# Two 64-row matmuls, one in each half of the array, for the low weights of the last 64 channels of product one

## What is computed

```python
w = np.exp(weight - weight.max(-1, keepdims=True)); w /= w.sum(-1, keepdims=True) + 1e-9
x = einsum('hk,bskhg->bshg', w, last_7_tokens(x_pad)).reshape(8192, 192)
h = x @ w_in_1;  x = (h / (1 + np.exp(-h))) @ w_out_1                      # layer one
h = x @ w_in_2;  out = np.where(h > 0, h, np.exp(np.minimum(h, 0)) - 1) @ w_out_2   # layer two
```

## Time and profile before

| | |
|---|---|
| median of the runs | 1193.97 us |
| span of the profiled execution | 1191.4 us |
| TensorE matmul busy | 1167.8 us, 98% |
| TensorE weight load busy | 964.3 us, 81% |
| VectorE busy | 880.6 us, 74% |
| ScalarE busy | 454.8 us, 38% |
| GpSimd busy | 64.9 us, 5%, all before 130 us |
| matmuls | 5130, of which 10 warm up |

### The profile page before, as it was taken

How to read it: one execution, slowest core, us unless ns; L and a number is a source line. 1 busy time by engine, 2 the same in 40 slices (tenths; PEclk the granted TensorE clock), 3 DMA queues, 4 the chain that set the end, 5 groups by cost and what they waited for, 6 DMA issues and landing times.

```text
span 1191.4 us, 12698 instructions
## 1 busy us (share of the span) xinstructions
PE 1167.8 (98%) x5130; PEld 964.3 (81%) x5130; DVE 880.6 (74%) x1023; ACT 454.8 (38%) x499; POOL 64.9 (5%) x57
## 2 busy tenths in 40 slices
PE   4999999999999999999999999999999999999998
PEld 3788888888888888888888888888888888888886
DVE  6999647679977745677997764676898775577676
ACT  5243334444423234444433232444443222354443
POOL 6444100000000000000000000000000000000000
PEclk8999999999999999999999999999999999999999
DMA  4321000000010000000100000000011000000000
GB/s 146 96 65 32 18 1 1 14 15 14 19 32 18 19 1 1 1 14 14 32 14 18 19 18 1 1 14 1 14 32 32 1 1 1 1 1 14 14 1 26
DMA packets 16843, 22.94 MB, mean 19 GB/s; under 512 B 1424, under 2 KB 9616, under 8 KB 16784
## 3 DMA queue, kind: packets, MB, share of 16 engines
q1 hardware_dynamic: 16784, 22.13, 6.2%
HBM read 15.83 MB, written 6.29 MB: 19 GB/s over the span
## 4 chain that ended last, share of the span: by engine, by line
PE 96%; DVE 3%; DMA 0%; issue 0%; ACT 0%; SPq 0%; ACTq 0%; DVEq 0%
PE hid L504 48%; PE acc L528 19%; PE acc L531 19%; PE acc L530 10%; DVE mix L375 1%; DVE mix L338 1%; DVE glo L429 1%; DMA xT<-x_rows 0%; DVE ghi L441 0%; DVE mix L371 0%; ACT ghi L291 0%; DVE mix L335 0%; DVE x L355 0%; DVE g L453 0%; ACT g L299 0%
## 5 line engine op out<-in xcount | busy, mean ns | idle before, releaser
L504 PE MATMUL hid<-x,wi 128*128 128x512 f32 x2560 | 623.1, 390 | 6.2 <-DVE x L355 6.2
L504 PEld LDWEIGHTS hid<-x,wi 128*128 128x128 f32 x2560 | 481.4, 188 | 106.8 <-DVE x L355 6.6
L299 ACT ACTIVATE g<-hid 128x1024 f32<-128x1024 f32 x256 | 263.4, 1029 | 712.0 <-PE hid L504 696.0
L429 DVE TENSOR_TENSOR glo<-g,ghi 128x1024 fp32r<-128x1024 f32 x256 | 319.1, 1247 | 31.7 <-ACT ghi L291 30.3
L441 DVE CAST ghi<-g 128x1024 fp32r<-128x1024 f32 x128 | 91.5, 714 | 150.5 <-ACT g L299 150.1
L528 PE MATMUL acc<-glo,wo 128*128 128x512 f32 x512 | 199.5, 390 | 2.5 <-DVE glo L429 2.5
L528 PE MATMUL acc<-ghi,wo 128*128 128x512 f32 x512 | 199.4, 390 | 1.2 <-ACT ghi L291 0.9
L531 PE MATMUL acc<-glo,wo 128*128 128x512 f32 x512 | 199.2, 389 | 0.0
L530 PE MATMUL acc<-ghi,wo 128*128 128x512 f32 x512 | 199.2, 389 | 0.0
L531 PE MATMUL acc<-ghi,wo 128*128 128x512 f32 x512 | 199.2, 389 | 0.0
L449 DVE TENSOR_SCALAR g<-g 128x1024 f32<-128x1024 f32 x128 | 88.7, 693 | 117.8 <-ACT g L299 117.2
(11 more groups left out here) (39 smaller groups left out, 212.6 us busy)
## 6 DMA issues: line engine op xcount, KB each, us to landing
xT<-x_rows SPq DMA_DIRECT2D x16, 518.0 KB, 4.2
stg<-w_in SPq DMA_DIRECT2D x16, 256.0 KB, 3.2
outT<-stg SPq DMA_DIRECT2D x16, 256.0 KB, 2.0
stg<-w_out SPq DMA_DIRECT2D x16, 192.0 KB, 3.3
outT<-tail SPq DMA_DIRECT2D x16, 128.0 KB, 2.3
tap<-tap_rows SPq DMA_DIRECT2D x1, 7.0 KB, 1.7
```

The costliest lines, as they stand in the source:

```text
L299: eng.activation(g[:, u % 2, :], hid[u % 2][:, :], fn).then_inc(s_fn, 1)
L429: eng.tensor_tensor(glo[:, u % NG, :], g[:, u % 2, :], ghi[:, u % NG, :].bitcast(F32), ALU.subtract).then_inc(s_glo, 1)
L504: last = eng.matmul(hid[u % 2][:, t * TOK:(t + 1) * TOK], w[:, j, wk, t * P:(t + 1) * P], xs[:, xk, :], start=n == 0, stop=n == len(plan) - 1)
```

## The change

The two full matmuls of the pair (3, 2) become two matmuls of 64 rows: tile t = 0 with the low weights on partitions 0 to 63, tile t = 1 with those on partitions 64 to 127. Both have the high part of x as the moving operand, which must therefore stand on both halves. A new tile `x1d` (layer one) or `x2d` (layer two) holds the second copy of it. For even chunks `x[:, 2]` has the high part on 0 to 63 and the copy lies on 64 to 127; for odd chunks it is the other way round, so that an even and an odd chunk share a copy tile.

```diff
-        wi = [sb(f"wi{l}", [P, NPAIR, 4, PW], F32R) for l in range(2)]
+        wi = [sb(f"wi{l}", [P, NPAIR, 3 * PW + P], F32R) for l in range(2)]
...
+        x1d = sb("x1d", [P, TOK], F32R)
+        x2d = sb("x2d", [P, GROUP // 2, TOK], F32R)
...
+        LOW, HIGH = slice(0, REST), slice(REST, P)
+
+        def hi_rows(c):
+            return HIGH if c % 2 else LOW
...
             def first_matmul(u):
...
-                plan = [(0, 0), (0, 1), (2, 0), (1, 2), (3, 2)]
+                plan = [(0, 0), (0, 1), (2, 0), (1, 2)]
                 for n, (wk, xk) in enumerate(plan):
...
                     for t in range(2):
-                        last = eng.matmul(hid[u % 2][:, t * TOK:(t + 1) * TOK],
-                                          w[:, j, wk, t * P:(t + 1) * P], xs[:, xk, :],
-                                          start=n == 0, stop=n == len(plan) - 1)
+                        eng.matmul(hid_t[t], w[:, j, wk * PW + t * P:wk * PW + (t + 1) * P], xs[:, xk, :],
+                                   start=n == 0, stop=False)
+                if c == 0:
+                    eng.wait_ge(s_wlo, POOL_OPS * (l * NPAIR + j) + 3)
+                for t, rows in enumerate((LOW, HIGH)):
+                    mv = xs[rows, 2, :] if rows == hi_rows(c) else xd[rows]
+                    last = eng.matmul(hid_t[t], w[rows, j, 3 * PW:3 * PW + P], mv, start=False, stop=True)
                 last.then_inc(s_hid, 1)
```

On GpSimd the one subtraction of a piece's input weights becomes three, and on VectorE one operation is added to the averaging of each chunk (19 steps for 18) and one to `split_result`:

```diff
-                eng.tensor_tensor(wi[l][:, j, 2:4, :].rearrange("p a n -> p (a n)"), stg_in(q),
-                                  wi[l][:, j, 0:2, :].rearrange("p a n -> p (a n)").bitcast(F32),
-                                  ALU.subtract).then_inc(s_wlo, 1)
+                eng.tensor_tensor(wi[l][:, j, 2 * PW:3 * PW], stg_in(q)[:, 0:PW],
+                                  wi[l][:, j, 0:PW].bitcast(F32), ALU.subtract).then_inc(s_wlo, 1)
+                for t, rows in enumerate((LOW, HIGH)):
+                    cols = slice(PW + t * P, PW + (t + 1) * P)
+                    if t:
+                        eng.wait_ge(s_wlo, POOL_OPS * q + 2)
+                    eng.tensor_tensor(wi[l][rows, j, 3 * PW:3 * PW + P], stg_in(q)[rows, cols],
+                                      wi[l][rows, j, cols].bitcast(F32), ALU.subtract).then_inc(s_wlo, 1)
...
-                eng.tensor_copy(xs[:, 2, :], tail[:, :]).then_inc(s_x2, 1)
-                eng.wait_ge(s_x2, 3 * rank(s) - 1)
-                eng.tensor_tensor(xs[REST:P, 2, :], tail[REST:P, :], xs[REST:P, 2, :].bitcast(F32),
-                                  ALU.subtract).then_inc(s_x2, 1)
+                eng.tensor_copy(xd[low], tail[low, :]).then_inc(s_x2, 1)
+                eng.tensor_copy(xs[high, 2, :], tail[high, :]).then_inc(s_x2, 1)
+                eng.wait_ge(s_x2, X2_OPS * rank(s) - 2)
+                eng.tensor_tensor(xs[low, 2, :], tail[low, :], xd[low].bitcast(F32), ALU.subtract)\
+                   .then_inc(s_x2, 1)
```

More of the change, by code:

```diff
@@ L81, in mixed_two_layer_ffn @@
     conv_start[1], conv_len[1] = 0, NPAIR - 2
-    CONV_OPS = 2 * NTAP + 4
+    CONV_OPS = 2 * NTAP + 5
+    POOL_OPS = 5
+    X2_OPS = 4
     POOL_TAPS = 5
@@ L187, in load_piece, with lo_rows, x_of, dup_of @@
                .then_inc(done, 16)
+        LOW, HIGH = slice(0, REST), slice(REST, P)
+        def hi_rows(c):
+            return HIGH if c % 2 else LOW
+        def lo_rows(c):
+            return LOW if c % 2 else HIGH
+        def x_of(l, c):
+            return x2[:, c % GROUP, :, :] if l else x1[:, c % 2, :, :]
+        def dup_of(l, c):
+            return x2d[:, c % GROUP // 2, :] if l else x1d[:, :]
         block = ctx.enter_context(nc.Block())
@@ L279, in _ @@
             eng.wait_ge(s_tap, 7)
[L280 to L283, removed]
+            eng.wait_ge(s_mix0, MIX0_STEPS - 1)
+            eng.activation(x1[:, 0, 0, :], mix[:, 0, :], ACT.Copy, scale=tstat[:, 4:5]).then_inc(s_hi0, 1)
+            eng.wait_ge(s_mix0, MIX0_STEPS)
+            eng.activation(x1d[HIGH, :], mix[HIGH, 1, :], ACT.Copy, scale=tstat[HIGH, 5:6]).then_inc(s_hi0, 1)
+            eng.activation(x1[LOW, 0, 2, :], mix[LOW, 1, :], ACT.Copy, scale=tstat[LOW, 5:6]).then_inc(s_hi0, 1)
             for q in range(2, NSTG):
@@ L350, in _ @@
             eng.wait_ge(s_tap, 7)
[L351 to L357, removed]
+            eng.wait_ge(s_hi0, 1)
+            eng.scalar_tensor_tensor(x1[:, 0, 1, :], mix[:, 0, :], tstat[:, 4:5], x1[:, 0, 0, :].bitcast(F32),
+                                     ALU.mult, ALU.subtract).then_inc(s_lo0, 1)
+            eng.wait_ge(s_hi0, 2)
+            eng.scalar_tensor_tensor(x1[HIGH, 0, 2, :], mix[HIGH, 1, :], tstat[HIGH, 5:6],
+                                     x1d[HIGH, :].bitcast(F32), ALU.mult, ALU.subtract).then_inc(s_lo0, 1)
             def conv_op(c, i):
@@ L366, in conv_op @@
                         eng.wait_ge(s_lo0, 2)
-                        eng.wait_ge(s_hi0, 2)
+                        eng.wait_ge(s_hi0, 3)
                     else:
@@ L377, in conv_op @@
                 else:
-                    xs = x1[:, c % 2, :, :]
+                    xs, xd = x_of(0, c), dup_of(0, c)
+                    high, low = hi_rows(c), lo_rows(c)
+                    r0, r1 = tstat[:, 4:5], tstat[:, 5:6]
                     if i == 2 * NTAP and c >= 2:
@@ L413, in split_result @@
             def split_result(s):
-                a, xs = acc[s % 2], x2[:, chunk(s) % GROUP, :, :]
+                c = chunk(s)
+                a, xs, xd = acc[s % 2], x_of(1, c), dup_of(1, c)
+                high, low = hi_rows(c), lo_rows(c)
                 eng.wait_ge(s_first1, rank(s))
@@ L493, in first_matmul @@
                         eng.wait_ge(s_fn, u - 1)
-                xs = x1[:, c % 2, :, :] if l == 0 else x2[:, c % GROUP, :, :]
-                w = wi[l]
-                plan = [(0, 0), (0, 1), (2, 0), (1, 2), (3, 2)]
+                xs, xd, w = x_of(l, c), dup_of(l, c), wi[l]
+                hid_t = [hid[u % 2][:, t * TOK:(t + 1) * TOK] for t in range(2)]
+                plan = [(0, 0), (0, 1), (2, 0), (1, 2)]
                 for n, (wk, xk) in enumerate(plan):
                     if c == 0 and n == 2:
-                        eng.wait_ge(s_wlo, 3 * (l * NPAIR + j) + 1)
+                        eng.wait_ge(s_wlo, POOL_OPS * (l * NPAIR + j) + 1)
                     if u == 0 and n == 3:
                         eng.wait_ge(s_lo0, 2)
+                        eng.wait_ge(s_hi0, 3)
                     for t in range(2):
-                        last = eng.matmul(hid[u % 2][:, t * TOK:(t + 1) * TOK],
-                                          w[:, j, wk, t * P:(t + 1) * P], xs[:, xk, :],
-                                          start=n == 0, stop=n == len(plan) - 1)
+                        eng.matmul(hid_t[t], w[:, j, wk * PW + t * P:wk * PW + (t + 1) * P], xs[:, xk, :],
[5 more added lines that the diff above has]
+                    last = eng.matmul(hid_t[t], w[rows, j, 3 * PW:3 * PW + P], mv, start=False, stop=True)
                 last.then_inc(s_hid, 1)
@@ L536, in _ @@
             eng.wait_ge(s_whi, 1)
[L537 removed]
+            warm = wi[0][:, 0, 0:TOK]
             for i in range(WARM):
```

32 lines of the change are left out of this document (18 added, 14 removed).

## The result

The changed kernel takes 1241.9 us, the median of 4 runs (1241.29 to 1242.03), against 1193.99 of before: 1.0401 times as long, with an interval of 1.0386 to 1.0416. The profiled execution has a span of 1239.5 us, 48.1 more than before. I had forecast 1151.5 and a range to 1228; it is 4% slower.

The account below looks back on a forecast made before the run. TensorE's matmul slots were taken to bound the kernel: 232 units x 0.2267 = 52.6 us saved, minus 7 and 3, left 42.6, so a span of 1148.8 and a median of 1151.5 us; range 1138 to 1228.

Parts of the forecast that it names:

- What bounds the kernel: Whole kernel: TensorE's 5,120 matmuls of 0.2267 us make 1160.5 of the 1191.4 us; VectorE stands close behind in some stages.
- I take 'together': Each unit's pair: loads hidden, both 64-row matmuls stream at once, 0.2267 us saved a unit, 52.6 in 232 units; chance 0.40.
- The row I leaned on: TensorE at 35.45 after a wait: an exposed weight load, the next load starting at 35.56, so 0.11 us a load.
- the emptying with loads held back: At each change of matmul form the array must empty and two loads a unit are exposed: 1275 us; chance 0.12.
- The variant with loads ahead: The array empties at each change of matmul form, 0.324 us paid a unit, but loads stay hidden: 1224 us; chance 0.18.
- My break-even: A pause of about 98 ns at each change between full and half matmuls, (52.6 - 7) / 464, decides gain or loss.
- The term of 7 us for stages 0 to 2: VectorE sets the pace there: stages 1 and 2 4.7 us longer, stage 0 2.7 longer, nothing saved in 24 units.
- the price of 0.37 us of VectorE for each microsecond of GpSimd: Stages 1 and 2: 11.2 us of VectorE lost to 30.3 of GpSimd; 15.0 more GpSimd means 5.6 more VectorE.
- Stages 7, 15 and 23: VectorE needs 35.9 us in stages that would be 34.45; 1 us each comes back as waits, 3 in all.
- 0.34 for slower: Chance given to the changed kernel being slower than before, against 0.61 for faster and 0.05 for the same.

Follow-up runs that it names:

- 19 slots: The changed kernel with one full matmul in place of the two half ones, one tile's low weights left out: 1136.78 us, 0.952 of before.
- the kernel with the cut alone: The kernel before, with GpSimd's 512-element subtraction cut by columns into 256, 128 and 128 and TensorE's wait split: 1190.71 us, 0.9975 of before.

## Why the prediction was wrong, point by point

**What bounds the kernel** was right: TensorE alone sets the steady stages, 36.27 then and 37.89 now. But "only fewer or shorter matmul slots, or a stall, can move the end" passed over the stretch ahead of the first product, 19.85 us long, at whose end TensorE waits for VectorE: the other engines' edits made it 1.4 us shorter, and the sum had no term for it.

**The step that failed** is "I take 'together'", with a load of 0.11 hidden in the slot before and nothing lost at the passage. The pair's loads do go out together (within 0.01 us) and the pair does share a slot, which the kernel with both halves on the same partitions shows. But the loads go out only 0.09 us after the slot of the full matmul ahead, 0.32 after its start, where a full load starts with it; and the next full load goes out in the same way behind the pair. That they wait for the array to empty is my reading of these times, and the short half matmuls, which leave both gaps as they are, agree with it. The row I leaned on the earlier trace rows gave the price of an exposed load rightly, 0.11. What it could not give is that both changes of form expose one.

**The rival that came true** is the emptying with loads held back, at 0.12, given 1275. Its mechanism is the measured one; its size was too high, because I took the empty stretch from the end of a matmul's record, 0.162, and it is 0.09. With the measured terms a unit loses 2 x (0.09 + 0.11) - 0.2267 = 0.17, and 0.03 by the lower pace behind; 256 x 0.203 = 52. Less the 2.4 gained elsewhere, some 1243.6 come out where 1241.9 was measured. The rest lies in stage 0, whose units wait for other things and don't lose 0.2 each: it takes 36.33 us here and 36.70 with full matmuls (granted clock 0.95 and 0.93), while the other 248 units at 0.203 make 50.3. Put into my own sum for this rival, the measured 0.09 gives 1193.97 + 232 x 0.173 + 7 = 1241.1. That this hits is luck: it leaves out the pace and has 7 us with the wrong sign. The variant with loads ahead (1224) is shown false by the late loads. My break-even, a pause of 98 ns at each passage, counted only a pause; the measured 0.09 lies under it, and the change still loses, because with the load it is twice 0.20 against 0.2267. The Trainium skill's sentence that a change of tiling mode drains TensorE (TensorEngine Tiling (Array Packing), Key Properties) agrees with these traces, at 0.09 us empty and 0.11 of load each time. Its other one, that a load whose row group doesn't conflict is pulled ahead (TensorE: Matmul & The Clock Gate, The mechanism), agrees between the halves: the pair's two loads start within 0.01 us, and so do its two matmuls. It says nothing of a half load behind a full matmul, which holds both halves. I weighed the second rule for a place that only the first one speaks of.

**VectorE and GpSimd.** The term of 7 us for stages 0 to 2 had the wrong sign. With full matmuls the other engines' changes gain 2.4; with 19 slots the three stages took 105.4 us, not 117. The step at fault is the price of 0.37 us of VectorE for each microsecond of GpSimd. It came from rows with one long operation a piece. GpSimd's time rose from 15.46 to 19.92 us in stage 1, and yet a tap fell from 1065 to 927 ns. The taps are held up less by three short operations than by one long one, as the kernel with the cut alone shows. That the two engines can alternate, each finding a gap, is my reading and not shown. The lengths of GpSimd's operations were off as well: 1.31 us for the one of 256 and 0.88 for each of 128, where I had 1.19 and 1.08, and those of the output weights fell to 0.97 and 0.89, so a piece takes 4.93 us, not 5.63. I also took VectorE's busy time as a demand of its stage, while what doesn't fit moves into the next: with one full matmul, stages 1 and 2 hold 68.9 us of its work, not 77.2, and stage 3 has 19.56 where it had 17.60.

**Stages 7, 15 and 23** were rightly seen as near the edge. When a unit was shorter, each cost 0.3 and the stage behind it 0.1, instead of 1: VectorE is busy 34.63 us of 34.78 in stage 7, and the rest of its work stands in stage 8, 30.62 where it was 29.30. In the changed kernel they cost nothing.

**The chances.** 0.34 for slower was too little for a step that no row showed and a rule spoke against; and the range left out the variant that came.

## What to carry to other kernels

A pair of 64-row matmuls in different halves of the array does share a slot. But a stream of full matmuls pays about 0.20 us to enter the form and 0.20 to leave it, nearly two slots of 512 columns, so it pays only where at least two pairs stand together, and by little even then (9.05 us for 9.07 of two units here). By an estimate from these numbers every further pair in the same phase would save a slot of 0.2267; no run here has more than two. Where a helper engine's long operations run beside a busy VectorE, cutting them short, with finer counts for those who wait, can be worth more than the operations it adds (1190.7 us for 1193.8 here); try it first, since it is easy to undo. A weight load that hides under one kind of matmul need not hide under another, so price it from the row where the kind changes, or give that rival a real chance.

## What the hardware showed that I had not expected

After a passage, and after two matmuls of 96 rows without any passage, the full matmuls that follow start 0.23 to 0.24 us apart instead of 0.2267, at an unchanged granted clock of 1.00. How long it lasts differs: five distances behind the pair of the changed kernel, ten behind one half matmul alone (a unit of 4.767 us against 4.74), eleven with 96 rows, where this is all that is lost, 0.06 us a unit. The same pace stands in the kernel before where TensorE resumes after a wait: from 35.79 on, behind the earlier trace rows, nine distances average 0.232. What causes it stays open; no run here separates it.
